# Routed experts on TensorE: 128 tokens per tile as the held operand, or the weights as the held operand with 288 tokens along the columns

## What is computed

```python
def _moe2_ref(x, w_gate, w1, w2):          # x: 2304 x 512, w1: 8 x 512 x 1024, w2: 8 x 1024 x 512
    logits = x @ w_gate
    expert_idx = np.argmax(logits, axis=1)
    ...
    for e in range(E):
        mask = expert_idx == e
        ...
        xe = x[mask]
        h = np.maximum(xe @ w1[e], 0.0)
        ye = h @ w2[e]
        out[mask] = gate_w[mask, None] * ye
```

## Time and profile before

| | |
|---|---|
| median of 3 runs | 836.25 us (835.97 to 838.12) |
| profiled execution, its own time | 836.29 us |
| its span, from the first to the last instruction | 834.2 us, so 2.1 us lie around it |
| mean granted TensorE clock | 0.995 |
| busy: PE, weight load, DVE, ACT, POOL | 95%, 83%, 46%, 36%, 35% |
| expert stage, first matmul to the last matmul's end | 568.5 to 822.5 us |

### The profile page before, as it was taken

One profiled execution on the slowest core, in us unless ns is written; L12 is line 12 of the kernel. 1 busy time (PEld: TensorE's weight loads), 2 busy tenths in 40 slices (PEclk: granted clock), 3 DMA queues, 4 the chain that ended last, 5 costly groups with the idle time before them and its releaser, 6 DMA issues.

```text
span 834.2 us, 16210 instructions
## 1 busy us (share of the span) xinstructions
PE 795.5 (95%) x4966; PEld 689.3 (83%) x4967; DVE 385.2 (46%) x920; ACT 302.9 (36%) x667; POOL 288.0 (35%) x255
## 2 busy tenths in 40 slices
PE   5899989999999999999999999999899999999993
PEld 5777778899889899989989988987688888888882
DVE  5767767411234424424424437447645255255321
ACT  3777776633322322242232232432133142242210
POOL 4677875035222212222222223390223123123110
PEclk9999999999999999999999999999999999999997
DMA  7876773011130020020020010501616116111110
GB/s 259 297 254 222 254 266 123 26 38 39 57 121 1 0 75 0 0 75 0 0 75 0 0 39 1 202 15 51 242 48 244 39 38 245 38 38 44 38 40 29
DMA packets 25244, 74.52 MB, mean 89 GB/s; under 512 B 3072, under 2 KB 3200, under 8 KB 25088
## 3 DMA queue, kind: packets, MB, share of 16 engines
q1 hardware_dynamic: 21856, 63.68, 21.6%
q0 software_dynamic: 3360, 10.49, 3.7%
HBM read 61.57 MB, written 13.11 MB: 90 GB/s over the span
## 4 chain that ended last, share of the span: by engine, by line
PE 72%; issue 9%; POOL 9%; DVE 4%; ACT 4%; DMA 1%; DVEq 0%; ACTq 0%; SPq 0%; POOLq 0%
PE pj L678 20%; PE nm L861 14%; PE nm L1318 13%; PE kv L861 7%; PE nm L1301 6%; PE pj L1301 6%; POOL gl L831 2%; POOL sqt L192 2%; POOL sqt L188 2%; POOL W L1102 1%; ACT feat L388 1%; PE pj L1329 1%; PE tr L1287 1%; PE kv L1329 1%; DMA qk<-in_qk_n 1%
## 5 line engine op out<-in xcount | busy, mean ns | idle before, releaser
L831 POOL TENSOR_TENSOR gl<-g,gh 128x384 fp32r<-128x384 f32 x96 | 101.3, 1058 | 295.8 <-ACT gh L696 295.8
L691 DVE TENSOR_TENSOR g<-pj,sg 128x384 f32<-128x384 f32 x96 | 53.5, 557 | 226.2 <-ACT sg L686 225.9
L686 ACT ACTIVATE sg<-pj 128x384 f32<-128x384 f32 x96 | 47.2, 492 | 252.8 <-PE pj L678 252.8
L678 PE MATMUL pj<-xh,win_h 128*128 128x384 f32 x384 | 129.5, 337 | 1.2 <-DVE xl L713 1.2
L678 PE MATMUL pj<-xh,win_l 128*128 128x384 f32 x384 | 129.4, 337 | 0.0
L678 PE MATMUL pj<-xl,win_h 128*128 128x384 f32 x384 | 128.9, 336 | 0.0
L1318 PE MATMUL nm<-W,hTh 128*128 (+1 forms) x320 | 100.8, 396 | 1.3 <-DVE hTl L1480 1.3
L678 PEld LDWEIGHTS pj<-xh,win_h 128*128 128x128 f32 x384 | 72.1, 188 | 5.2 <-DVE xl L713 1.5
L678 PEld LDWEIGHTS pj<-xl,win_h 128*128 128x128 f32 x384 | 72.1, 188 | 3.6
L678 PEld LDWEIGHTS pj<-xh,win_l 128*128 128x128 f32 x384 | 72.0, 188 | 0.0
L1318 PEld LDWEIGHTS nm<-W,hTh 128*128 128x128 f32 x320 | 58.6, 188 | 13.0 <-issue 1.6
(11 more groups left out here) (240 smaller groups left out, 1542.2 us busy)
## 6 DMA issues: line engine op xcount, KB each, us to landing
wraw<-in_moe_w SPq DMA_DIRECT2D x7, 2048.0 KB, 8.7
ve<-in_v_z SPq DMA_DIRECT2D x16, 585.0 KB, 3.8
qk<-in_qk_n SPq DMA_DIRECT2D x16, 576.0 KB, 5.0
qkT<-in_qk_t SPq DMA_DIRECT2D x16, 576.0 KB, 5.3
y_rows<-ys SPq DMA_DIRECT2D x18, 256.0 KB, 2.3
stage<-in_moe_w_in SPq DMA_DIRECT2D x8, 512.0 KB, 6.0
y_early<-ys SPq DMA_DIRECT2D x12, 256.0 KB, 2.7
stage<-in_moe_w_out SPq DMA_DIRECT2D x4, 512.0 KB, 6.2
```

The source lines that it names most:

```text
L678: mm = eng.matmul(ph[f % 3][:, 0:BT], w[f // F1A][:, c, f % F1A, :], x[:, c, :], start=(c == 0 and w is win_h and x is xh), stop=(c == DC ...
L686: eng.activation(sg[f % 2][:, :], ph[f % 3][:, 0:BT], ACT.Sigmoid, scale=1.702).then_inc(a_sg, 1)
L691: eng.tensor_tensor(g32[f % 2][:, :], ph[f % 3][:, 0:BT], sg[f % 2][:, :], ALU.mult).then_inc(v_g, 1)
L831: eng.tensor_tensor(gl[f % 3][:, :], g32[f % 2][:, :], gh[f % 3][:, :].bitcast(F32), ALU.subtract).then_inc(g_gl, 1)
```

## The change

The roles in the experts' matmuls are swapped. A tile is now 288 tokens (`TOK`) of one expert in three parts of 96 (`SUB`, `SUBS`). `up` holds 128x128 pieces of w1 and streams the 288 token columns: 8 outputs of 128 hidden units, each 4 x 3 = 12 matmuls. The hidden values come out already lying as `down` needs them, so `turn_h` is gone; `down` holds pieces of w2, again 4 x 8 x 3 = 96 matmuls of 288 columns, and its output is features by tokens, so it is copied by ACT (`leave`) and turned back by `turn_y`, three groups of 4 transposes, before `result`. `turn_x` is four groups of 3 transposes, spread through `down` of the tile before. With 576 tokens in each of four experts there are 8 tiles, 1536 matmuls and 192 transposes, where there were 960 and 240.

`W` has one place. The next expert's w1 is split (ACT, then POOL, all four chunks) while `down` of the last tile of an expert runs, and w2 while the next `up` runs. DVE splits no weights after the first expert. The tile loop counts to 8 and enters a second loop only if there are more tiles. The first tile's gather is now three indirect DMAs, and it stands at step 13 of the last dense block instead of 9, since its buffers `xb` overlay data that the logit products read until then. `turn_x` of the first tile is spread over the end of the dense layer.

```diff
-FIRST = 2
-TILES = (N + FIRST * P + E * (P - 1)) // P
-SLOTS = 2
+SUB, SUBS = 96, 3
+TOK = SUB * SUBS
+TILES = (N + TOK + E * (TOK - 1)) // TOK
...
-    W = at("W", [P, SLOTS, 4, EW], 53248, F32R)
+    W = at("W", [P, 4, EW], 53248, F32R)
...
-            if f == 9:
-                eng.wait_ge(*dense["early"])
-                gather(eng, 0)
             if f == 13:
-                low(eng, 0, 0, 1, 0)
+
+                eng.wait_ge(*dense["product"])
+                eng.wait_ge(*dense["early"])
+                gather(eng, 0)
...
+        def up(eng, t, k, after):
+
+            for j in range(F2):
+
+                need(eng, v_h, F2 * t + j - 2)
+                for c in range(DC):
+                    if j == 0:
+                        eng.wait_ge(lo[0], CHUNKS * k + c + 1)
+                        eng.wait_ge(v_tx, DC * t + c + 1)
+                    for w, x in ((HI, xTh), (HI, xTl), (LO, xTh)):
+                        mm = eng.matmul(ph[j % 3][:, 0:TOK], weights(w[0], c * FF2 + j * P), x[:, c, :],
+                                        start=(c == 0 and w is HI and x is xTh), stop=(c == DC - 1 and w is LO))
+                mm.then_inc(p_hh, 1)
+                if j in after:
+                    after[j]()
...
+        def turn_y(eng, t, s):
+            if s == 0:
+                eng.wait_ge(a_yt, DC * t + DC)
+            need(eng, v_o, SUBS * t + s)
+            for d in range(DC):
+                mm = eng.transpose(pt[0:SUB, d * P:(d + 1) * P], yTs[:, d, s * SUB:(s + 1) * SUB], ident[:, :])
+            mm.then_inc(p_ty, 1)
...
+            def body(t):
+                gather(eng, t + 1)
+                if isinstance(t, int):
+                    beside_tile(eng, t - 1, lambda k: lows(eng, k, 0))
+                beside_tile(eng, t - 1, lambda k: lows(eng, k, 1))
+                scatter(eng, t - 1)
+                beside_tile(eng, t, lambda k: lows(eng, k, 0))
```

More of the change, by code:

```diff
@@ L1210, in after @@
-            def after(last):
-                scatter(eng, last)
-                eng.wait_ge(st_o, 16 * last + 16)
-            tiles(eng, first, second, body, after)
+                beside_tile(eng, t, lambda k: lows(eng, k, 0))
+            body(1)
+            tiles(eng, last, body)
+            scatter(eng, last)
+            for s in range(SUBS):
+                eng.wait_ge(st_o[s], 16 * last + 16)
         return ahead, late
@@ L1413, in late @@
-            tiles(eng, first, second, body, lambda last: None)
+            for j in range(F2):
+                high_h(eng, 0, j)
+                if j == 3:
+                    eng.wait_ge(v_dl, 1)
+                    eng.activation(ex[:, :, :], dl[:, :, :], ACT.Exp).then_inc(a_ex, 1)
+            leave(eng, 0, 0)
+            leave(eng, 0, 1)
+            high_x(eng, 1, 0)
+            leave(eng, 0, 2)
+            high_x(eng, 1, 1)
+            high_x(eng, 1, 2)
+            leave(eng, 0, 3)
@@ L1659, in late @@
-            tiles(eng, first, second, body, lambda last: result(eng, last))
+            eng.wait_ge(*dense["logits"])
+            choose(eng, T_L, pick_l)
+            eng.sem_inc(v_dl, 1)
+            low_h(eng, 0, 0)
+            eng.wait_ge(p_cn, 2)
+            link(eng, eng.tensor_tensor(tot[:, :], pr[:, PR_TOTAL:PR_TOTAL + E], adj[:, :], ALU.add))
+            ranked(eng, T_L, pos_l)
+            link(eng, eng.scalar_tensor_tensor(out=rank[:, T_L], in0=oh[:, 0, T_L], scalar=adj[:, 0:1],
+                                               in1=rank[:, T_L], op0=ALU.mult, op1=ALU.add))
@@ new lines, in late @@
+            link(eng, eng.scalar_tensor_tensor(out=head[:, :], in0=tile, scalar=float(P), in1=row1,
+                                               op0=ALU.mult, op1=ALU.add))
+            link(eng, eng.tensor_scalar(gid[:, :], head[:, :], -1.0, 0.0, ALU.add, ALU.max))
+            rows(eng, 1, gid, SUBS)
+            gating()
+            table()
+            low_x(eng, 1, 0)
+            eng.wait_ge(g_v, 4)
+            spread(V_GATE, V_GATE + 1)
+            low_x(eng, 1, 1)
+            spread(V_GATE + 1, V_GATE + 2)
@@ new lines, in late @@
+            low_x(eng, 1, 2)
+            spread(V_GATE + 2, VALS).then_inc(v_val, 1)
+            low_x(eng, 1, 3)
+            tokens()
+            eng.wait_ge(y_done, 16 * NT)
+            last = last_tile(eng)
+            def body(t):
+                rows(eng, t + 1, gid, SUBS * (t + 1))
+                for j in range(F2):
+                    low_h(eng, t, j)
+                    if j == 0 and isinstance(t, int):
+                        gate_values()
+                    if j % 2 and j // 2 < SUBS:
+                        result(eng, t - 1, j // 2)
+                for c in range(DC):
+                    low_x(eng, t + 1, c)
@@ L1661, in vector @@
+            body(1)
+            tiles(eng, last, body)
+            for s in range(SUBS):
+                result(eng, last, s)
         return ahead, late
-    CONSTANTS = 14
+    CONSTANTS = 15
     return {"sync": sync(), "gpsimd": gpsimd(), "tensor": tensor(), "scalar": scalar(), "vector": vector()}
```

633 lines of the change are left out of this document (273 added, 360 removed).

## The result

| | before | changed kernel |
|---|---|---|
| median of the runs | 836.12 us (835.97 to 838.12, 4 runs) | 822.09 us (821.01 to 823.42, 4 runs) |
| span of the profiled execution | 834.2 us | 819.4 us (its own time 821.22) |
| ratio of the two | | 0.983, 95% interval 0.980 to 0.985 |

The change gains 14 us. The forecast was 816 us with a range of 805 to 828: the sign and the range held, the value was 6 us too low. In the profiled executions the span came out at 819.4 us where the sum gave 814.0.

A forecast was written before the change was run, and what follows sets the result against it. TensorE's own work was taken as the bound. 834.2 + 5.4 (first gather) + 1.7 (clock) - 28.5 (expert stage) + 1.2 (end) = 814.0 us span; with 2.1 around it, 816 us forecast, range 805 to 828.

The forecast's parts named there:

- the 821 of a rival: Start of the expert stage: first tile-1 gather or inversion late by 2 to 8 us, total 821 us; chance 17%.
- the landing of the third gather: First tile's rows: third DMA issued by about 559.6, landing near 562.0, so TensorE stands 4.9 us at `turn_x`.
- The clock's term: Behind the 4.9 us wait at the first `turn_x`: TensorE's clock falls to half, costing 1.7 us, between 0 and 3.9.
- nothing else is late behind the hole: After TensorE's wait at first `turn_x`: nothing is late any more, and the earlier 0.43 us wait for `gl` goes.
- The line through 384 and 512 columns: Expert matmuls: 173.4 ns at 384 columns and 229 at 512 give 131.7 ns at 288; 131.3 taken.
- the prediction's second reading: Transposes per tile: if load costs, the 12 holding 96 columns take 82 ns instead of 109, saving 0.3 us.
- the same floor: TensorE's matmuls: 109 ns is a floor set by loading the held operand, beside the stream; 288 columns lie above it.
- The pace of 149 ns: Expert matmuls of 288 columns: load and stream interfere, 149 ns each, +27.5 us, total 843; rival's chance 7%.
- the ninth tile: Expert stage: one token across a boundary makes a ninth tile, +27.8 us, total 844; rival's chance 2%.
- The refill: Expert switches: POOL's chunks at 4.8 instead of 2.4 us make w1 and w2 late, +49, total 865; rival's chance 4%.
- `low_h`, `low_x` and `result` all read PSUM, so it leaves my sum as it is: Expert stage: DVE and POOL block each other on SBUF, but DVE with one SBUF input doesn't contend; nothing added.
- No hole: First `turn_x`: rows land sooner or the clock stays, total 809 to 812 us; chance 15%.

The follow-up runs named there:

- the early gather: Changed kernel with the first tile's gather issued at step 10 of the last dense block instead of 13, POOL's weight chunks at steps 9, 11, 15, 15: 813.99 us.

## Why the prediction was right in the main and 6 us off

The median of 822.1 lies in the range, but outside the 813 to 819 that the prediction gave its own account, and next to the 821 of a rival whose cause did not come: behind the first expert matmul the start took no longer than laid out. So the range is right by its width, and the sum is short in several terms that all err the same way.

The difference in span, 819.4 - 814.0, parts into three places that sum to it.

**Up to the first expert matmul, +2.1 us** (577.66 against 573.9 + 1.7). The step that failed is the landing of the third gather, put at 562.0 and measured at 564.45. Three terms of it were mis-sized: the issues stand 1.28 to 1.49 us apart, not 1.03, because 0.3 us lie between two of them; the chunk ahead of them took 3.38 us because DVE got a second chunk in that step, which the prediction laid out nowhere (1.1 us, by the experiment that put them apart); and 0.8 us had been lost earlier, in code that is the same in both kernels. That is a difference between executions and no cost of the change: the first matmul of the dense layer starts at 155.39 before and at 155.95 now, and between 154.50 and 156.91 in the traces of the experiments. Against that the stretch behind the wait was shorter than summed. (The prediction's rows add up to 5.3 rather than its 5.4.) The clock's term was near, 1.7 forecast and 1.5 to 1.6 measured, with some luck: it was picked between 0 and 3.9 for a hole of 4.9 us, the hole was 6.4, and one of 5.28 cost 2.2. That nothing else is late behind the hole was right too, as the early gather shows. What was missing is the thought that followed from the mechanism: a gather that waits for the last `logit_pair` only needs those that read the memory under `xb`, and they were done three steps earlier.

**First to last expert matmul, +1.6 us** (227.1 against 225.5). A tile took 28.07 us against 27.8, 2.2 us in all: the pace was 133.3 ns against 131.3, 0.4 us a tile. The line through 384 and 512 columns has a slope of 0.434 ns a column, and from 384 to 288 it is 0.418; the cost beside the stream is constant at 13 ns rather than shrinking. The transposes gave back 0.3 us a tile, the amount of the prediction's second reading, but by luck. It had those that hold 96 columns at 82 ns, because of the load; these are `turn_y`, and they take 110. The twelve of `turn_x` stream 96 columns and hold 128, and they take 83. So a transpose costs by what it streams or by the rows that it holds, which these two shapes don't tell apart, and not by the columns that it holds: its 109 ns was no sign of the same floor. The switches cost 0.1 us each instead of 0.3, reading the tile table cost one stall of 0.72 that wasn't in the sum, and the waits of the start came out 0.7 shorter than laid out.

**Behind the last matmul, +1.7 us** (14.6 against 12.9). The third scatter starts 7.15 us after the last matmul; the sum set this start against the end of the one of before (0.9 us mis-sized). And leaving the loop of empty tiles was put at 3.3 us, but from the last scatter's end to the span's end it is 6.55 us now and was 8.76: 2.2 came back. What of that loop had run beside something else that still has to end was not tried.

**The rivals.** The pace of 149 ns, the ninth tile and the start of 821 us didn't come. The refill was not late, with 1.9 us to spare for w1 (the chunks end at 690.7, `up` starts at 692.56), near the 2.2 forecast. But the step "`low_h`, `low_x` and `result` all read PSUM, so it leaves my sum as it is" was incomplete: the copies of row numbers do not, and they are what fails first, and hardest, when POOL gets longer. *No hole* was counted as an outcome of chance, 809 to 812 us. It is a choice in the code, and with it the kernel takes 814.0.

**Where the 14 us come from.** Per token the new tile isn't faster: 28.07 us for 288 is 97.5 ns, and 12.30 us for 128 was 96.1. The gain is that 20 x 128 = 2560 columns became 8 x 288 = 2304, for the 2304 tokens that there are, 10% of 246 us. By the traces these 256 columns are 24.6 us, the dearer token takes 3.2 back, TensorE's other waits between the first and the last expert matmul are 5.5 us fewer (2.5 against 8.0), and the later first matmul (9.15) and the longer end (2.9) leave 14.8 of span. No experiment takes these terms apart; they are intervals of the two traces.

## What to carry to other kernels

Cost a wider or turned tile per useful token, not per matmul. Here a token's columns cost no less than before, and what was won on them is padding that went. The same turning with a tile of 192 tokens would cost 192 x 112 / 192 = 112 ns of `up` and `down` a token, where 288 cost 192 x 133.3 / 288 = 89: at 192 columns the floor of 112 ns sets the pace, at 256 not yet.

Where a DMA's issue is moved behind other work on its engine, take its landing from the last issue with the gaps between issues, and look for the earliest point at which its memory is really free. Here that was worth 8 us.

Slack on GpSimd is shorter than its own timeline says when VectorE has a small SBUF-to-SBUF copy in the path; put such copies on another engine.

## What the runs showed that I had not expected

- A 96x3 copy on DVE was held for 17.17 us beside a row of POOL's `tensor_tensor` instructions, against 0.17 alone, and the same copy on ACT took 0.19.
- TensorE recorded as busy for all of 590 to 610 and 690 to 700 us had its clock at half when each matmul streamed 96 columns.
- In one trace each, a hole of 5.28 us cost 2.20 us of clock and one of 6.40 us cost 1.48. The price of the clock doesn't follow the length of the hole.
- A wait of 2.96 us for `gl` left the clock at 1.00.
